# Another order of ScalarE's and VectorE's instructions in the h stage of a gated layer

## What is computed

```python
h = np.maximum(x @ w_in, 0.0)                    # (B, 768, 1024)
hp = pad h with one zero token on either side
conv_out = sum(conv_w[k][None, None, :] * hp[:, k:k + S, :] for k in range(3))
gate = 1.0 / (1.0 + np.exp(-conv_out))
return (h * gate) @ w_out                        # (B, 768, 320)
```

## Time and profile before

| | us |
|---|---|
| median of 3 runs | 895.04 |
| lowest and highest run | 893.45, 900.79 |
| the profiled execution | 894.39 |
| its span | 892.7 |
| PE (TensorE matmul) busy | 793.6 (89%) |
| DVE (VectorE) busy | 507.4 (57%) |
| ACT (ScalarE) busy | 389.8 (44%) |
| POOL (GpSimd) busy | 290.0 (32%) |

### The profile page before, as it was taken

One profiled execution on the slowest core, in us unless ns is written; L12 is line 12 of the kernel. 1 busy time (PEld: TensorE's weight loads), 2 busy tenths in 40 slices (PEclk: granted clock), 3 DMA queues, 4 the chain that ended last, 5 costly groups with the idle time before them and its releaser, 6 DMA issues.

```text
span 892.7 us, 29938 instructions
## 1 busy us (share of the span) xinstructions
PE 793.6 (89%) x13477; PEld 732.7 (82%) x13477; DVE 507.4 (57%) x706; ACT 389.8 (44%) x521; POOL 290.0 (32%) x476
## 2 busy tenths in 40 slices
PE   4776998999988998787899998999989999899997
PEld 4765887888877887676779998999989999899997
DVE  5794664575656653322348468534775347753485
ACT  1222334334343434334456186622757127561374
POOL 4078884880861865800012200212002020030200
PEclk9796889989999997979999999999999999999999
DMA  9996964885695554443160010100101001010001
GB/s 113 140 136 113 119 108 93 105 121 110 87 134 95 87 130 87 136 83 77 35 189 1 1 36 18 45 1 1 37 18 45 1 2 35 18 44 1 1 1 44
DMA packets 238203, 59.10 MB, mean 66 GB/s; under 512 B 228448, under 2 KB 233468, under 8 KB 238076
## 3 DMA queue, kind: packets, MB, share of 16 engines
q1 hardware_dynamic: 160092, 43.75, 25.5%
q10 hardware_dynamic: 77984, 13.45, 11.1%
HBM read 43.01 MB, written 14.16 MB: 64 GB/s over the span
## 4 chain that ended last, share of the span: by engine, by line
PE 56%; DVE 12%; POOL 10%; ACT 9%; issue 8%; DMA 3%; ACTq 2%; SPq 1%; DVEq 0%; POOLq 0%
PE p L1045 26%; PE p L690 11%; DVE stage L1332 6%; PE p L848 3%; POOL y_t L442 3%; PE p L788 3%; ACT big L1237 3%; DVE big L1251 3%; POOL prod L439 3%; POOL t_pair L459 2%; PE p L1137 2%; PE p L798 2%; PE p L814 2%; PE p L833 2%; POOL prod L456 2%
## 5 line engine op out<-in xcount | busy, mean ns | idle before, releaser
L1347 POOL TENSOR_TENSOR big<-stage,big 128x1024 fp32r<-128x1024 f32 x12 | 28.8, 2397 | 287.6 <-DVE stage L1287 287.6
L1045 PE MATMUL p<-xs,w 128*128 128x384 f32 x560 | 110.5, 336 | 5.8 <-ACT tmp L1225 5.8
L456 POOL TENSOR_TENSOR prod<-t_pair 128x30 f32<-128x30 f32 (+9 forms) x150 | 84.2, 561 | 85.9 <-DMA t_pair<-m_scratch 74.4
L1045 PEld LDWEIGHTS p<-xs,w 128*128 128x128 f32 x560 | 98.4, 188 | 7.2 <-ACT tmp L1225 6.9
L1045 PE MATMUL p<-wo,big 128*128 128x320 f32 x576 | 93.9, 321 | 9.2 <-DVE big L1251 9.1
L459 POOL TENSOR_TENSOR t_pair<-t_pair,prod 128x30 f32<-128x30 f32 (+9 forms) x150 | 97.1, 647 | 11.7
L1045 PEld LDWEIGHTS p<-wo,big 128*128 128x128 f32 x576 | 89.8, 197 | 12.6 <-DVE big L1251 11.2
L1045 PE MATMUL p<-wsg_hi,big 128*128 128x384 f32 x384 | 98.5, 335 | 0.9 <-ACT stage L1199 0.6
L1045 PEld LDWEIGHTS p<-wsg_hi,big 128*128 128x128 f32 x384 | 69.6, 188 | 1.9 <-ACT stage L1199 1.2
L1332 DVE SCALAR_TENSOR_TENSOR stage<-tmp,cols,stage 128x768 f32<-128x768 f32 x48 | 48.4, 1016 | 12.9 <-ACT stage L1229 12.0
L1209 ACT ACTIVATE big<-tmp 128x768 fp32r<-128x768 f32 x16 | 13.6, 847 | 95.5 <-DVE tmp L1307 95.5
(11 more groups left out here) (154 smaller groups left out, 1678.0 us busy)
## 6 DMA issues: line engine op xcount, KB each, us to landing
raw_r<-in_r_dram SPq DMA_DIRECT2D x48, 80.0 KB
vp<-in_v_dram ACTq DMA_DIRECT2D x96, 40.0 KB, 2.3
x_scratch<-y_t ACTq DMA_DIRECT2D x48, 80.0 KB
out_dram<-stage SPq DMA_DIRECT2D x11, 320.0 KB, 2.3
m_scratch<-n_t SPq DMA_DIRECT2D x48, 64.0 KB, 2.6
t_pair<-m_scratch SPq DMA_DIRECT2D x5, 512.0 KB, 5.0
t_scratch<-t_pair SPq DMA_DIRECT2D x5, 512.0 KB, 3.3
t_sb<-t_scratch SPq DMA_DIRECT2D x20, 128.0 KB, 2.7
```

The source lines that it names most:

```text
L456: pool.tensor_tensor(p_v, tp[:, 0:s, s:s + 1].to_broadcast([PAIRS, s, n]), tp[:, s:s + 1, s + 1:C].to_broadcast([PAIRS, s, n]), ALU.mult). ...
L1045: last = pe.matmul(out_of(p, half), l, r, start=step == 0 and first, stop=step == steps - 1 and not part)
L1347: pool.tensor_tensor(dst, src, hi.bitcast(F32), ALU.subtract).then_inc(sem_, 1)
```

## The change

One round now finishes more of a tile. On ScalarE: tap f, high part f-1, Relu f+1 (in the last round the move of the next batch's first x tile), sigmoid f. On VectorE: product f-1, taps f (after the last tile, the low part of the next x), low part f-1. No instruction is added or taken away; all waits are for the same results as before.

```diff
-                for f in range(F2 + 2):
+                def take_h(f):
+                    p, free = wait_full(act, b, ("h", f))
...
+                    if f >= 3:
+                        act.wait_ge(h_mul, b * F2 + f - 2)
+                    act.activation(as_two(hp[f % 3][:, 1:S + 1]), two(p, P, HS), ACT.Relu).then_inc(free, 1)
+
+                take_h(0)
+                for f in range(F2 + 1):
                     if f < F2:
-                        p, free = wait_full(act, b, ("h", f))
...
-                        act.activation(as_two(hp[f % 3][:, 1:S + 1]), two(p, P, HS), ACT.Relu).then_inc(free, 1)
                         wait_taken(act, b, ("h", f))
                         if f >= 3:
                             act.wait_ge(h_lo, b * F2 + f - 2)
                         act.activation(cv[:, f % 3], hp[f % 3][:, 0:S], ACT.Copy, scale=taps[:, 0, f:f + 1]).then_inc(h_tap, 1)
-                    if 1 <= f <= F2:
-                        act.wait_ge(h_conv, (b * F2 + f) * 2)
-                        act.activation(cv[:, (f - 1) % 3], cv[:, (f - 1) % 3], ACT.Sigmoid).then_inc(h_sig, 1)
-                    if f == F2 and b + 1 < B:
+                    if f >= 1:
+                        act.wait_ge(h_mul, b * F2 + f)
+                        act.activation(hg[:, 0, f - 1, :], cv[:, (f - 1) % 3], ACT.Copy).then_inc(h_hi, 1)
+                    if f + 1 < F2:
+                        take_h(f + 1)
+                    elif f < F2 and b + 1 < B:
                         take_x(b + 1, 0)
-                    if f >= 2:
-                        act.wait_ge(h_mul, b * F2 + f - 1)
-                        act.activation(hg[:, 0, f - 2, :], cv[:, (f - 2) % 3], ACT.Copy).then_inc(h_hi, 1)
+                    if f < F2:
+                        act.wait_ge(h_conv, (b * F2 + f + 1) * 2)
+                        act.activation(cv[:, f % 3], cv[:, f % 3], ACT.Sigmoid).then_inc(h_sig, 1)
...
-                for f in range(F2 + 2):
-                    if f >= 2:
-                        dve.wait_ge(h_hi, b * F2 + f - 1)
-                        low(hg[:, 1, f - 2, :], cv[:, (f - 2) % 3], hg[:, 0, f - 2, :], h_lo)
+                for f in range(F2 + 1):
+                    if f >= 1:
+                        k = (f - 1) % 3
+                        dve.wait_ge(h_sig, b * F2 + f)
+                        dve.tensor_tensor(cv[:, k], cv[:, k], hp[k][:, 1:S + 1], ALU.mult).then_inc(h_mul, 1)
                     if f < F2:
                         k = f % 3
                         dve.wait_ge(h_tap, b * F2 + f + 1)
...
-                    if 1 <= f <= F2:
-                        k = (f - 1) % 3
-                        dve.wait_ge(h_sig, b * F2 + f)
-                        dve.tensor_tensor(cv[:, k], cv[:, k], hp[k][:, 1:S + 1], ALU.mult).then_inc(h_mul, 1)
-                    if f == F2 and b + 1 < B:
+                    elif b + 1 < B:
                         low_x(b + 1, 0)
+                    if f >= 1:
+                        dve.wait_ge(h_hi, b * F2 + f)
+                        low(hg[:, 1, f - 1, :], cv[:, (f - 1) % 3], hg[:, 0, f - 1, :], h_lo)
```

More of the change, by code:

```diff
@@ L1215, in _ @@
                 act.activation(g.warm[:], cols[:, 0:1], ACT.Sigmoid)
-                for f in range(F2 + 2):
-                    if f < F2:
-                        p, free = wait_full(act, b, ("h", f))
[L1219 to L1224, removed]
-                        act.activation(as_two(hp[f % 3][:, 1:S + 1]), two(p, P, HS), ACT.Relu).then_inc(free, 1)
+                def take_h(f):
+                    p, free = wait_full(act, b, ("h", f))
+                    if f == 0 and b == 0:
+                        act.wait_ge(edge, 2)
+                    if f == 2:
+                        act.wait_ge(edge, b + 3)
+                    if f >= 3:
[3 more added lines that the diff above has]
+                for f in range(F2 + 1):
+                    if f < F2:
                         wait_taken(act, b, ("h", f))
```

## The result

The changed kernel takes 885.33 us (median of 4 runs, 883.71 to 886.48) against 895.13 us (4 runs): the ratio is 0.988, with a 95% interval of 0.983 to 0.993. It is faster by 1.2%, and 885.33 lies inside the stated range, 0.1 us from the forecast. That it is as near as 0.1 us is luck: by the medians the gain is 9.80 us where 9.04 were forecast, and single runs of the kernel before lie up to 7 us apart (893.45 to 900.79). Run a second time beside the kernel before, it gave a ratio of 0.989 (0.983 to 0.996). The profiled execution after took 886.48 us with a span of 884.8, against 894.39 and 892.7 before.

The account below looks back on a forecast made before the run. TensorE was taken to set most of the pace, with an early and a late pause from VectorE and ScalarE. Gains of 0.69 + 2.84 + 2.85 + 2.66 = 9.04 us took 894.39 to 885.35; range 883.6 to 889.6.

Parts of the forecast that it names:

- What bounds the stage: h stage before: TensorE sets most of the pace, with pauses of 1.46 us before h(5) and 1.82 or 2.42 before y(6).
- The start becomes slower: Start of the h stage: new TensorE pauses of 1.28, 0.96 and 1.12 us before h(4), y(0), h(5); h(5) 1.70 late.
- The round of 3.86 us: VectorE and ScalarE, first tiles: sigmoid, handover, product and taps in series take 3.86 us a round, against 4.72 before.
- the rival of 0.14 each: VectorE-ScalarE handovers up to h(5): each costs 0.14 us, 3.4 us in all, giving 888.7; no chance of its own.
- TensorE the bound from h(5) on, low parts with 2 us to spare: From h(5) to v: only TensorE's work, 26.89 us; low parts 6 and 7 some 2 us early, late pause gone.
- the last rival: TensorE's pauses only move from the end of the h stage to the beginning, giving 894.4; chance 0.04.
- The term of 1.36 us in each of three batches: End of the h stage, y(6) to v: the low clock behind the late pause costs 1.36 us, saved by the change.
- The rival by which it falls at the end of the stage anyway: The clock falls there for a reason other than the pause; 4.1 us of gain go, giving 889.4; chance 0.05.
- The rival by which the clock falls in the new pauses: Start of the h stage: the clock falls at the three new pauses, once a batch, giving 890.8; chance 0.06.
- The rival's price: Price of each clock fall in the new pauses at the start of the stage: 1.36 us a time.
- the rival of two falls a batch: h stage: the clock falls at h(4) and again later, 8 x 1.36 = 10.9 us, giving 896.2; chance 0.03 (or worse).
- The sum: Gains over the four batches' h stages: 9.04 us in all, 885.35 from the profiled execution's 894.39.

Follow-up runs that it names:

- early_relu: Changed kernel with the Relus of tiles 2 to 5 one round earlier and those of tiles 6 and 7 ahead of the high part: 869.09 us.
- act_only: Changed kernel with VectorE's loop put back to the order of before, so only ScalarE's order is new: 931.86 us.
- dve_only: Changed kernel with ScalarE's loop put back to the order of before, so only VectorE's order is new: 913.52 us.
- late_pause5: Changed kernel with five small extra VectorE instructions, results unused, ahead of low part 6 in each batch: 890.28 us.
- late_pause7: Changed kernel with seven small extra VectorE instructions, results unused, ahead of low part 6 in each batch: 900.61 us.
- long_early: Changed kernel with two small extra VectorE instructions, results unused, ahead of the taps of tiles 0, 1 and 2: 894.94 us.
- relu2_only: Changed kernel with only the Relu of tile 2 moved forward, behind the Relu of tile 1 and ahead of sigmoid 0: 887.21 us.

## Why the prediction was right

**What bounds the stage.** Right: TensorE's work sets the pace but for places that ScalarE and VectorE set. "Everything between is back to back" was read too coarsely. The row of 54 matmuls in the earlier trace rows takes 8.34 us, some 0.26 more than three y tiles need without a wait (13.36 for the five of the changed kernel, less two of 2.64): low part 5 ended at 878.69, 0.1 us after y(5) could have started. The sum does not change by this, since it goes by starts.

**The start becomes slower.** Forecast: h(4), y(0), h(5) start 6.86, 10.72 and 14.58 us after h(2). Measured: 6.89, 10.75 and 14.60 in the last batch. The mechanism, a Relu queued behind a high part that waits for a product, is shown by `early_relu`, which moves only Relus and loses all three pauses.

**The round of 3.86 us.** Measured 3.86. Its pieces were taken from rows in another order, with handovers at the lower part of their bounds; they measure 0.03, so the rival of 0.14 each is out. That the round needs both halves is shown by `act_only` (6.10) and `dve_only` (5.45).

**TensorE the bound from h(5) on, low parts with 2 us to spare.** Right: no pause, and the chain above runs over TensorE alone. Low parts 6 and 7 in the changed kernel, last batch:

```profile
872.46 0.95 DVE L1256 TENSOR_TENSOR big<-stage,big 128x768 fp32r<-128x768 f32 x1
875.33 0.96 DVE L1256 TENSOR_TENSOR big<-stage,big 128x768 fp32r<-128x768 f32 x1 [0.91 <-ACT big L1235]
```

They end at 873.41 and 876.29, and y(6) and y(7) start at about 875.71 and 878.34: 2.3 and 2.05 us to spare, where 2.2 and 1.9 were forecast. `late_pause5` and `late_pause7` measure the same room by filling it. From h(4) to v they take 36.24 and 37.71 us, 1.58 and 3.05 more than the changed kernel's 34.66. The two further instructions thus cost 1.47, 0.73 each; five are 3.6 us, of which 1.4 came out (y(6) starts 37.66 us after h(2), 36.26 in the changed kernel). The rest, 2.2 us, was room. That the pauses only move from the end to the start, the last rival, is out with this.

**The clock.** The fall was real in batches 0 and 1 of before as well, which the earlier trace rows did not show:

```profile
555.26 7.08 PE L1045 MATMUL p<-wo,big 128*128 128x320 f32 x36 [2.42 <-DVE big L1251]
664.90 7.08 PE L1045 MATMUL p<-wo,big 128*128 128x320 f32 x36 [2.42 <-DVE big L1251]
```

```profile
555.00:559.00 4.00, 3.74 (x15) 3.74 (x16) 3.96 (x6) 2.31 (x3) 0.00 (x0) 0.58 0.00 0
665.00:669.00 4.00, 4.00 (x17) 4.00 (x18) 3.96 (x5) 2.31 (x3) 0.00 (x0) 0.59 0.00 0
```

In windows of 1 us the granted clock of the kernel before is 0.50 over 556 to 559, 665 to 668 and 775 to 777, and 1.00 again from 560, 669 and 778; the profiles give both levels only as shares of the full clock. The 6.73 us of the forecast are those of batch 2, where the earlier trace rows have the clock at 0.57. The term of 1.36 us in each of three batches was right in sum, with its parts a little off. Without a fall y(6) to v takes 5.49 us behind a pause (`late_pause7`), not 5.37: the restart there is 0.19 us and not 0.11 (5.30 without a pause, from the 13.20 us between the starts of y(3) and v in batch 0 of the changed kernel, 547.06 to 560.26). So the clock cost 1.43, 1.44 and 1.24 us in batches 0 to 2, 4.11 in all, where 4.08 were forecast. That the long pause is the cause is borne out by all the runs together: from h(2) on, no fall in an h stage of the ten profiles stands anywhere but at a pause of 2.18 us or more, and such pauses had one in most batches (2.18 in `dve_only`: two of four; 2.26: three of four; 2.42: three of three; 2.49: three of four; 2.67: two of four). Behind 1.21 us it fell in none of four, and behind 1.82 not in the one batch that had it. `late_pause5` and `late_pause7` alone, none and two of four, would be too few to show it. The rival by which it falls at the end of the stage anyway is out: with the pause gone, it stayed at 1.00 there in all eight stages.

That it fell in all three batches of before with a pause of 2.42, though, was not certain: in `late_pause7` a longer pause failed to bring it down twice. So of the 9.0 us, the 4.1 of clock are the profiled execution's; another run of the kernel before may pay a different number of falls. The batches of one run that differ with the same pause show it too (2.67 us in `late_pause7`: two of four; 2.26 or 2.27 us in `long_early`: three of four). The rival by which the clock falls in the new pauses did not come true: three pauses of 1.2, 0.8 and 0.9 us near each other brought no fall in eight stages.

**The rival's price** was mis-sized where no run tested it before: a clock that falls ahead of y(0) costs 0.44 us or less, not 1.36 (`relu2_only`, `long_early`), because TensorE then waits ahead of h(5) anyway. That holds for the rival of two falls a batch as well: its 896.2 took both at the full price. Its remark that ten more falls would bring over 1% is also off; at 1.36 us each, slower by 1% is (9.04 + 8.95) / 1.36, some 14 falls in all, six more than its eight.

**The sum.** 885.35 for the profiled execution, 886.48 measured. Of the 1.13 us, 0.83 lie ahead of the first h stage (h(2) of batch 0 at 518.70, before 517.87), which the change doesn't touch, and 0.27 in three stages of 41.56 in place of 41.47. The last batch gained 0.68 from h(2) to the end of the span (45.35 us, before 46.03), forecast 0.69. So the sum for the four stages is right by its mechanism. What lies ahead of them differs by up to 6.6 us between the profiles (513.26 to 519.90), and it is luck that the two compared here are only 0.83 apart.

## What to carry to other kernels

These are drawn from this one kernel. Where two in-order engines hand a tile back and forth, reorder them as a pair, and write down the round for both: with VectorE's or ScalarE's half alone this kernel was 20 and 38 us slower than before (913.52 and 931.86 against 893.39 on that chip). Place an instruction that frees a buffer for the bounding engine ahead of one that waits for a third engine, for every tile of the start-up chain: all of them gained 14.8 us (`early_relu`), the first alone only moved the pause (`relu2_only`). Where the bounding engine is TensorE, price a long pause (here those of 2.18 us or more) with the clock that may fall behind it (1.41 us in `late_pause7`), but only if the work behind it is on the path.

## What the runs showed of the hardware

An equal pause of TensorE (2.67 us) brought its clock to a lower level, 0.50 of the full one in windows of 1 us (559 to 561 in batch 0), in two of four batches of one execution, `late_pause7`; pauses of 3.96 us (`act_only`, ahead of h(4)) did so in all four, 1.21 us in none. What the lower level then cost was 1.41 us in `late_pause7`, up to 2.63 us in `dve_only` where it lasted longer, and nothing in `long_early` up to h(5), where TensorE had a wait behind it (h(5) 17.59 us after h(2), fall or no fall).
